# Beta moved out of the keys of a chunked delta-rule recurrence, two remainders laid out block-diagonally, and the queues written in a new order

## The reference

```python
def _attn_ref(q, k, v, beta):          # B, H, S, D = 4, 8, 768, 48
    k_n = k / (np.linalg.norm(k, axis=-1, keepdims=True) + 1e-06)
    state = np.zeros((B, H, D, D), dtype=np.float32)
    y = np.zeros_like(q)
    for t in range(S):
        kt, vt, bt = (k_n[:, :, t], v[:, :, t], beta[:, :, t, None])
        y[:, :, t] = np.einsum('bhd,bhde->bhe', q[:, :, t], state)
        v_old = np.einsum('bhde,bhd->bhe', state, kt)
        state = state + bt[:, :, :, None] * np.einsum('bhd,bhe->bhde', kt, vt - v_old)
    return y
```

## Time and profile before

| what | us |
|---|---|
| median of 3 runs | 893.18 (891.72 to 897.72) |
| the profiled execution, its own time | 890.49 |
| its span, first to last instruction | 888.8 |
| TensorE busy (matmul) | 834.0 |
| VectorE busy | 581.9 |
| ScalarE busy | 440.8 |
| GpSimd busy | 312.0 |

### The profile page before, as it was taken

How to read it: one execution, slowest core, us unless ns; L and a number is a source line. 1 busy time by engine, 2 the same in 40 slices (tenths; PEclk the granted TensorE clock), 3 DMA queues, 4 the chain that set the end, 5 groups by cost and what they waited for, 6 DMA issues and landing times.

```text
span 888.8 us, 31663 instructions
## 1 busy us (share of the span) xinstructions
PE 834.0 (94%) x13800; PEld 764.1 (86%) x13800; DVE 581.9 (65%) x1116; ACT 440.8 (50%) x833; POOL 312.0 (35%) x366
## 2 busy tenths in 40 slices
PE   2888999998999999899999999999999999999998
PEld 2677777777777777779999999999999999999997
DVE  6887889888888888757616426346465835646534
ACT  5776777767666766447124124234344333334221
POOL 7784768786757673204100000000012121121220
PEclk9999999989999999999999999999999999999999
DMA  8113121112121200301000000001410100100101
GB/s 294 59 45 121 34 64 40 58 33 63 34 63 35 63 25 22 119 4 54 1 0 1 1 0 0 0 1 63 168 37 1 55 1 1 53 0 0 54 1 54
DMA packets 21680, 38.25 MB, mean 43 GB/s; under 512 B 1840, under 2 KB 15664, under 8 KB 21552
## 3 DMA queue, kind: packets, MB, share of 16 engines
q1 hardware_dynamic: 21552, 36.35, 12.4%
HBM read 31.56 MB, written 4.72 MB: 41 GB/s over the span
## 4 chain that ended last, share of the span: by engine, by line
PE 85%; issue 5%; DVE 5%; ACT 3%; POOL 1%; DMA 1%; SPq 0%; ACTq 0%; DVEq 0%; POOLq 0%
PE dense_ps L1101 16%; PE dense_ps L1102 16%; PE dense_ps L1103 16%; PE t_ps L872 4%; PE front_ps L836 4%; PE z_ps L881 4%; PE t_ps L859 3%; PE t_ps L868 3%; PE front_ps L823 3%; PE side_ps L939 2%; PE side_ps L981 2%; PE extra_ps L993 1%; PE t_ps L848 1%; PE side_ps L964 1%; PE extra_ps L898 1%
## 5 line engine op out<-in xcount | busy, mean ns | idle before, releaser
L1303 POOL TENSOR_TENSOR vn_f<-vn_f 128x384 f32<-128x384 f32 x24 | 24.5, 1021 | 393.7 <-ACT vn_f L1348 393.7
L1102 PE MATMUL dense_ps<-w_spatial_pair,vn_pair 128*128 128x384 f32 x336 | 112.3, 334 | 0.0
L1101 PE MATMUL dense_ps<-w_spatial_pair,vn_pair 128*128 128x384 f32 x336 | 112.3, 334 | 0.0
L1103 PE MATMUL dense_ps<-w_spatial_pair,vn_pair 128*128 128x384 f32 x336 | 112.3, 334 | 0.0
L674 DVE TENSOR_TENSOR w_more<-t_ps,ident_band_lower 64x256 f16<-64x256 f32 x192 | 80.3, 418 | 17.7 <-PE t_ps L859 14.8
L461 ACT ACTIVATE t<-t_ps 128x512 f16<-128x512 f16 (+1 forms) x144 | 59.9, 417 | 38.1 <-PE t_ps L872 35.4
L1544 DVE TENSOR_TENSOR vn_pair<-vn_f,vn_pair 128x384 fp32r<-128x384 f32 x48 | 31.7, 662 | 58.7 <-ACT vn_pair L1310 58.7
L1103 PEld LDWEIGHTS dense_ps<-w_spatial_pair,vn_pair 128*128 128x128 f32 x336 | 63.1, 188 | 0.0
L1102 PEld LDWEIGHTS dense_ps<-w_spatial_pair,vn_pair 128*128 128x128 f32 x336 | 63.1, 188 | 0.0
L1101 PEld LDWEIGHTS dense_ps<-w_spatial_pair,vn_pair 128*128 128x128 f32 x336 | 63.1, 188 | 0.0
L1480 DVE BATCH_NORM_STATS2 stats<-v_u_f 128x6 f32<-128x512 f32 x24 | 16.7, 694 | 62.6 <-ACT v_u_f L1368 62.4
(11 more groups left out here) (228 smaller groups left out, 2643.7 us busy)
## 6 DMA issues: line engine op xcount, KB each, us to landing
qT_in<-in_q SPq DMA_DIRECT2D x24, 256.0 KB, 3.7
k_in<-in_k SPq DMA_DIRECT2D x24, 192.0 KB, 3.4
v_in<-in_v SPq DMA_DIRECT2D x24, 192.0 KB, 2.4
outT<-g_f SPq DMA_DIRECT2D x6, 576.0 KB, 3.3
w_spatial_f<-in_w_spT SPq DMA_DIRECT2D x3, 768.0 KB, 7.2
w_in_f<-in_k SPq DMA_DIRECT2D x3, 576.0 KB, 7.3
x_f<-in_k SPq DMA_DIRECT2D x3, 576.0 KB, 9.5
w_in_f<-in_w_in SPq DMA_DIRECT2D x1, 1536.0 KB, 7.8
```

The costliest lines, as they stand in the source:

```text
L1101: mm(out, lhs(LO), rhs(HI), start=first, stop=False)
L1102: mm(out, lhs(HI), rhs(LO), start=False, stop=False)
L1103: return mm(out, lhs(HI), rhs(HI), start=False, stop=last)
```

## The change

Beta no longer enters the keys. GpSimd multiplies the mask for N by beta of each row position (`scaled_masks`, from rows of beta that a DMA spreads over 64 partitions, two more DMAs for each unit), and multiplies the right side of the solve by beta (`r_scaled`). So there is one set of keys: one flip of 8 transposes, one copy by ScalarE, and `key_betas`, `beta_rests` and the beta high part go. The rests of N and of z are block-diagonal like `n_diags`: `newton` uses 8 whole-array matmuls for 16 quarter ones, `solve` 8 for 16. GpSimd makes the rest of N in two halves, ScalarE copies the rest of z in two. The f16 copy `n_highs` goes and `z_odd` reads the f32 mask product instead. The rest of the queries goes from VectorE to GpSimd, behind one more scaling copy on ScalarE (`q_scale`). Zeros of eight tiles are written by DMAs at the start instead of by VectorE. All queues have a new order, and one stage (`turn_x` and what hangs on it) moves to the following body, so that the loops go two bodies further.

```diff
-KB, KQ, AS, NS_, ZS, TS = 7, 6, 5, 4, 4, 3
+KB, KQ, AS, NS_, ZS, TS = 6, 6, 5, 4, 4, 3
...
+    mb = copies("mask_beta", 2, [P, 2, H, C])
...
-    nh = copies("n_high", NS_, [P, H, C], F16)
-    kbp = copies("kb_pair", KB, [P, 2, H, C], F16)
+    nl = copies("n_rest", 2, [P, H, P], F16)
+    knp = copies("kn_pair", KB, [P, 2, H, C], F16)
...
-    zl = m.sb("z_rest", [P, H, C], F16)
+    zl = m.sb("z_rest", [P, H, P], F16)
...
-    bodies = range(-4, NU + 3)
+    bodies = range(-4, NU + 5)
...
+        def beta_load(u):
+            need(sp, na_masked, 2 * (u - 1))
+            for i, r in enumerate(SIDES):
+                sp.dma_start(mb[u % 2][r:r + C, 0].rearrange("p h c -> p (h c)"), rows_dram[u, i].partition_broadcast(C))\
+                    .then_inc(mb_in[u % 2], 16)
...
+        def query_rests(u):
+            pool.wait_ge(q_high, u + 1)
+            tt(kq[u % KQ][:, 1, :, 1, :], qf[u % 2][:], kq[u % KQ][:, 0, :, 1, :], ALU.subtract).then_inc(q_rest, 1)
...
+            pool.wait_ge(mb_in[u % 2], 32 * (u // 2 + 1))
+            tt(mb[u % 2][:, 0], cast(masks[:, 0], H), mb[u % 2][:, 0], ALU.mult).then_inc(mb_made, 1)
...
+                pool.wait_ge(r_second, n_carried(u + 1))
...
+            tt(rf[:], r, beta_of(u, D), ALU.mult).then_inc(r_ready, 1)
...
-        def z_rests(u):
+        def z_rests(u, r):
...
-            copy(zl[:], whole_(extra)).then_inc(zl_ready, 1)
+            copy(zl[r:r + C, :, r:r + C], whole_(extra)[r:r + C]).then_inc(zl_ready, 1)
...
             for h in range(H):
-                for r in SIDES:
-                    last = mm(tile(extra, r, h), nl[u % NS_][r:r + C, h, :], t[u % TS][r:r + C, h, :],
-                              start=False, stop=True, skip_group_check=True)
+                last = mm(extra[:, h * C:h * C + C], nl[u % NS_][:, h, :], t[u % TS][:, h, :],
+                          start=False, stop=True, skip_group_check=True)
...
             for h in range(H):
-                for e, (a, x) in enumerate(((zl, 0), (z[u % ZS], 1), (z[u % ZS], 0))):
+                mm(side[:, h // HP, h % HP * P:h % HP * P + D], zl[:, h, :], rp[:, h, 0],
+                   start=h % HP == 0, stop=False, skip_group_check=True)
+            for h in range(H):
+                for x in (1, 0):
                     for r in SIDES:
-                        last = mm(slot(h // HP, r, h % HP, False), a[r:r + C, h, :], rp[r:r + C, h, x],
-                                  start=e == 0, stop=e == 2)
+                        last = mm(slot(h // HP, r, h % HP, False), z[u % ZS][r:r + C, h, :], rp[r:r + C, h, x],
+                                  start=False, stop=x == 0, skip_group_check=True)
...
         def state(u):
-            pe.wait_ge(y_out, u + 1)
+            pe.wait_ge(u_rest, u + 1)
```

More of the change, by code:

```diff
@@ L739, in vector @@
         nc.vector.tensor_scalar(beta_up[:], beta, UP, None, ALU.mult).then_inc(beta_ready, 1)
-        for a in kbp[4:]:
-            clear(a[:].rearrange("p a h d -> p (a h d)"))
-        query(0)
-        for a in nd:
-            clear(a[:].rearrange("p h c -> p (h c)"))
+        dve.wait_ge(halves_in, 32)
+        for a in mb:
+            nc.vector.tensor_copy(a[:, 1], cast(masks[:, 1], H)).then_inc(beta_ready, 1)
         norm_sums(1)
         for j in bodies:
-            x, y, n, v, f, g = j, j - 1, j - 2, j - 3, j + 1, j + 2
+            x, y, n, v, f = j, j - 1, j - 2, j - 3, j + 1
+            if live(y):
+                level_z(y, 0)
+            if live(v):
+                u_rests(v)
+            if live(y):
+                level_w(y, 1, 0)
+                level_w(y, 1, C)
+            if live(v) and updates(v):
+                s_full(v)
+            if live(x):
+                mask(x, 1)
+            if x == 0:
+                norms(1, range(5))
+                norm_sums(2)
+                norm_sums(3)
+            if x == 1:
+                norm_sums(5)
+            if live(n):
+                level_w(n, 4, C)
+                level_z(n, 3)
+                level_w(n, 4, 0)
+            if live(v):
+                y_full(v)
             if live(y):
@@ L750, in vector @@
                 level_w(y, 2, C)
-            if live(n):
-                r_full(n)
+            if y == 0:
+                norm_sums(6)
+            if y == 2:
+                norms(2, (3,))
+            if live(n) and carries(n):
+                r_firsts(n)
+                r_seconds(n)
             if live(y):
                 level_z(y, 1)
-            if live(n) and carries(n):
-                r_second(n)
+            if y == 1:
+                norms(2, (0,))
             if live(n):
@@ L994, in turn_x @@
             last.then_inc(x_prod, 1)
-        pe.wait_ge(consts_half, 1)
+        pe.wait_ge(consts_made, 1)
         for j in bodies:
-            x, y, n, f, g = j, j - 1, j - 2, j + 1, j + 2
+            x, y, n, v, f, g = j, j - 1, j - 2, j - 3, j + 1, j + 2
             if live(y):
-                level_w(y, 2)
-            if live(n):
-                level_t(n, 4)
-            if live(n) and carries(n):
-                old_keys(n)
-            if live(x):
-                first_t(x)
+                level_z(y, 1)
             if live(n):
@@ L1020, in tensor @@
             if n == NU - 1:
-                values(1)
+                values(2)
+            if live(f):
+                products(f, 0)
             if live(y):
+                level_w(y, 3)
                 level_z(y, 2)
-                level_w(y, 3)
             if live(x):
```

479 lines of the change are left out of this document (239 added, 240 removed).

## The result

The changed kernel takes 899.22 us (median of 20 runs, 892.51 to 912.18) against 891.85 us (20 runs, 885.21 to 897.72): a ratio of 1.0082, interval 1.0055 to 1.011. The forecast was 880.9 us, and its range ended at 899. The profiled execution took 896.09 us with a span of 894.3 us, where before had 890.49 and 888.8.

A forecast was written before the change was run, and what follows sets the result against it. TensorE was taken as the bound, VectorE second. A body went 15.01 - 0.67 + 0.2 = 14.54 us; 22 bodies gave -10.3, with start and end -12.3: 878.2 profiled, 880.9 us forecast, range 871 to 899.

The forecast's parts named there:

- TensorE: right: TensorE's steps per body: flip -0.45, `newton` -0.22, `solve` +0.20, fewer passages to quarter matmuls -0.15; sum -0.62 us.
- The stalls: TensorE's stalls without a releaser, about 1.0 us a body: 0.05 us taken off for 5% fewer instructions.
- I keep its median: VectorE's `r_rests`, seen between 0.56 and 1.60 us beside GpSimd, priced at its old median, 1.09 us.
- the 0.2 us for the new waits: TensorE's waits in the new order, for `y_full`, `mask(f,0)`, `state` and others: 0.2 us a body, between 0 and 0.7.
- the waits eat the saving: Rival, chance 0.23: VectorE's in-order work from `r_firsts` to `mask(f,0)` adds 0.7 us a body; 893 us.
- the one I cited: Skill rule: GpSimd shares SBUF interfaces with VectorE's two-SBUF-input instructions; moving the query's subtraction takes one collision off each body.
- GpSimd: right, and not the bound: GpSimd's work per body, 10.2 to 11.7 us plus 1.4 idle before `z_odd`, still under a body of 14.3.
- Start and end: Outside the steady bodies: start -1.5 us with first products at 15, last three bodies -0.5 us.
- the 22 shorter bodies: Some 22 bodies taken as bound like the steady ones, each 0.47 us shorter: -10.3 us.

The follow-up runs named there:

- e5: Kernel before the change, plus 48 small VectorE memsets ahead of `r_rests` in four heaps of 12: 912.98 us, ratio 1.0166.
- e7: Changed kernel plus one wait: GpSimd starts `a_rests` only when `r_rests` is done: 886.52 us, ratio 0.9925.
- e3: Changed kernel with `s_rests` moved behind the next body's `level_w(y, 1)`, away from GpSimd's four operations: 907.53 us, ratio 1.0121.
- e6: Kernel before the change, plus 48 small VectorE memsets, two ahead of `r_rests` in every body: 898.29 us, ratio 1.0005.
- e2: Changed kernel with `win_rests` moved from the end of GpSimd's body into its wait before `z_odd`: 890.14 us, ratio 0.9945.
- e8: Changed kernel with `win_rests` moved ahead of `z_odd` and `a_rests` waiting for `r_rests`: 885.21 us, ratio 0.9911.
- e10: e8 with `z_even` and `x0_rests` moved between `r_scaled` and GpSimd's wait, and `n_rests` waiting for the masks: 887.23 us, ratio 0.9897.
- e1: Changed kernel with the copy `z_even` placed between `a_rests` and `scaled_masks`, and `n_rests` waiting for the masks: 899.15 us, ratio 1.0057.

## Why the prediction was wrong

**TensorE: right.** Steps of quiet bodies in the timeline of after, where `newton` runs from 308.40 to 309.09 and `solve` from 160.73 to 161.65:

```profile
305.78 0.62 PE L867 MATMUL front_ps<-identh,kn_pair 128*128 128x128 f16 x8
306.24 0.40 PE L902 MATMUL t_ps<-t,n_diag 128*128 128x64 f16 x8
...
308.40 0.38 PE L934 MATMUL extra_ps<-t,neg_ident 128*128 128x512 f16 x1
...
309.09 0.38 PE L921 MATMUL z_ps<-z,identh 128*128 128x512 f16 x1
...
160.73 0.37 PE L979 MATMUL side_ps<-rl_pair,z_rest 128*128 128x48 f16 x8
161.03 0.69 PE L984 MATMUL side_ps<-rl_pair,z 64*64 64x48 f16 x32
161.65 0.23 PE L924 MATMUL z_ps<-z,w 128*128 128x64 f16 x2
```

A flip is 0.46 us (forecast 0.45), `newton` 0.69 (0.70), `solve` 0.92 (near 0.9). TensorE's busy time for a body went from 13.71 (the seven bodies from 241.3 to 346.4 us of before) to 104.41 / 8 = 13.05: -0.66, where -0.62 was forecast. That quiet bodies gained 0.95 and not 0.66 goes with fewer stalls without a releaser: 5.6 us in eight bodies, against 8.1 in seven, or 0.46 a body; waits for other engines (1.3 us in the eight) take a part of that back.

**The stalls: not as treated.** I took 0.05 off them, for fewer instructions. From 89 to 340 us they are 16.7 us in before, 10.7 in after, 11.4 in e5, and 20.6 in e7. In these four traces they are small where TensorE waits for other engines (12.5 us in after, 11.3 in e5) and large where it doesn't (1.0 in before, 2.8 in e7), as if a wait of TensorE were partly paid by them and a saving on TensorE partly went to them. The other traces follow only roughly: e3 has 13.8 us of stalls beside 17.8 of waits, e6 13.9 beside 3.5. What makes the stalls, no run tested.

**VectorE, "I keep its median": this is the step that failed**, with the 0.2 us for the new waits that rests on it: the body of after is 15.14 us, 0.80 above the 14.34 that it would be without new waits, and in e7, without the collision, 0.31 above. `r_rests` was priced at 1.09 with 1.60 as its worst, both from rows in which GpSimd's order and phase were those of before. In after the usual one is better (0.61) and the bad one is 3.75 us, on five kinds of evidence: the timelines, e2 (other phase, no long ones, 1.4% faster), e3 (another phase, more of them, no faster), e5 (four delays of this size at this place alone make before 1.7% slower), and e7 (the wait that forbids the collision takes the ratio from 1.0082 to 0.9925). My rival "the waits eat the saving" had the right place and a price of 0.7 us in every body; in truth most bodies pay nothing, and a few pay 2 us of pause and more behind it at the lower clock. The clock's part stands in no term of mine, although show a granted clock of 0.98, and I could have asked what had lowered it.

The rows of after agree with a rule of the Trainium skill that says more than the one I cited. SBUF — State Buffer, section SBUF: two separate sides, says that the port pair which the two engines share is an exclusive lock: whichever starts first keeps it for the whole instruction and the other blocks fully. Two pairs show this. `s_rests` began at 311.34 inside `scaled_masks` (310.97 to 312.56) and ended 0.40 us after it. In e7 `a_rests` starts 0.15 us behind `s_rests` and is the one that is stretched, 1.41 for 1.16, while `s_rests` keeps 0.54. The Trainium skill speaks there of one instruction of the winner and not of who comes next; here `r_rests` waited through four, three of which started while VectorE was already waiting. The upper end of the term should have been GpSimd's run without a gap, 4.7 us in the long body (from 140.09, where `a_rests` starts, to 144.80, where `z_even` ends), and more with `key_rests` behind it, as e3's 4.88 us show.

**GpSimd: right, and not the bound.** Its rows in after:

```profile
L455 POOL TENSOR_TENSOR mask_beta<-mask,mask_beta 128x512 f32<-128x512 f32 x19 | 28.5, 1500 | 0.0
L392 POOL TENSOR_TENSOR n_rest<-na,n_diag 64x512 f16<-64x512 f32 x19 | 22.2, 1168 | 1.7 <-POOL kn_pair L442 1.7
...
L446 POOL TENSOR_TENSOR kq<-qT_in,kq 128x512 f16<-128x512 f32 x12 | 13.9, 1157 | 0.0
...
L417 POOL TENSOR_TENSOR z<-na,ident_band_lower 128x256 f16<-128x256 f32 x18 | 12.2, 677 | 38.9 <-DVE na L715 38.9
```

Half of the partitions costs all of the time (1.168 us), r_scaled 0.83, the query's rest 1.157, all as taken; only `scaled_masks` is 1.50 for 1.16, of which 0.23 is the collision (1.266 in e7). Busy time is 227.4 / 285 x 15.14 = 12.1 us a body, 11.7 was forecast, and there is idle time before `z_odd`. The step of exactly 8 bytes in `z_odd` costs nothing: 0.677 against 0.673.

**Start and end.** The first flip of the steady stretch stands 1.1 us earlier, near the -1.5 taken; the first products ran at 15.86, where 15 was forecast. The end is a second term that failed: 3.6 us longer in after and 2.9 in e7, where -0.5 was forecast, and three of the 22 shorter bodies (-1.4) lie there too. Of the 17.8 us between the forecast for the trace (-12.3) and the trace (+5.5), the 19 bodies have 11.3, the end 5.5, the start 0.4 and the other layers 0.6. What was seen in the end: in e7 TensorE waits 0.6 us there for the second copy of z's rest, 0.7 for `yf`, and stalls 4.6 us where before has 3.0, with the clock at 0.94 for 0.97. (The new order may have moved the flip a little within its body, so the border of the steady part is soft by a few tenths.)

**What the change is worth by itself.** In e7 the collision is out, and the result is 0.75% faster (0.4 to 1.1), 6.7 us where 12.3 were forecast; between the two traces it is only 3.2 us (885.6 against 888.8). Its body is (339.7 - 61.4) / 19 = 14.65 us against the 14.54 forecast, so the body was nearly right and 2 us of the difference are there; the rest is the end, and the start, whose gain is gone in e7 (61.4 for the 60.1 of after). The lowest ratios of the study are those of e8 and e10, the change with that wait and a fuller gap: 0.9911 and 0.9897, ahead of both kernels; from each other and from e7 their intervals do not part them.

## What to carry to other kernels

When work moves to GpSimd, look at every VectorE operation with two SBUF inputs that runs beside it, and bound it by the longest run of GpSimd operations without a gap, not by the median or the worst of the old trace; if such an operation is what TensorE waits for, let GpSimd wait for it (one line, worth 1.6% here), or move other work so that the two meet at a better point (1.4% here), as long as GpSimd has idle time elsewhere. Price a pause of TensorE of over 2 us at more than its length (1.3 to 1.7 times in e5) and look at the granted clock behind it, while the same delay in small pieces in slack costs nothing. A change that is right in every TensorE step can still lose by the phase between two other engines, and moving six small operations can win it back.

## What was not expected of the hardware

VectorE can lose not one but several boundaries in a row to GpSimd: three in after (3.75 us for 0.54), five in e3 (4.88, with the copy and `key_rests`), while GpSimd's operations keep their undisturbed 1.15, 1.27 and 0.82 us. Whether it gets in at the first boundary goes with how much of GpSimd's operation is left when VectorE arrives. In the six traces without the wait, every `r_rests` between 40 and 360 us that came with 0.28 us or less of `a_rests` to go got in behind it (310.81 to 311.01, say), and all 14 that came with 0.31 or more did not and took 2.17 to 4.88 us (140.72 to 141.24). At `scaled_masks` it is otherwise: with 0.84 to 1.13 us to go `r_rests` got in behind it (ten times), with 0.24 to 0.83 (six times) and with 1.16 (once) it did not, and `s_rests` got in with 1.2. What decides, no run isolates; this stays open.

Every pause of 2.1 to 3.0 us at `solve` in after and e5 came with 7 to 10 us at a granted clock of 0.50; in e3 it was 3 to 10. Stalls of 2.5 to 3.9 us without a releaser came with 3 to 7 us of it, and pauses of over 2 us in the first 40 us, where TensorE often stood idle (2.10 at 35.0 in e1, 2.27 at 35.4 in e7), with none. Four pauses at `solve`, put into the kernel before, cost 1.66%; 48 memsets spread out cost 0.05%, which is nothing that can be measured.
